# Attention on 128 partitions of four tokens and 32 of two: 1024-byte loads, turns of two tokens of a head, half-height score tiles and three softmax steps

## The reference

```python
# q, k, v: (4, 8, 576, 64)   p: (4, 8, 32, 64)
def sm_attn(qq, kk, vv):
    s = scale * np.matmul(qq, kk.transpose(0, 1, 3, 2))
    s = s - np.max(s, axis=-1, keepdims=True)
    a = np.exp(s)
    a = a / (np.sum(a, axis=-1, keepdims=True) + 1e-09)
    return np.matmul(a, vv)
p_packed = sm_attn(p, k, v)
out = sm_attn(q, p_packed, p_packed)
# then x = out as (2304 tokens, 512); P = gates of x; sum over 8 experts e of
# P[:, e] * (relu(x @ w1[e]) @ w2[e]); then (s * relu(x @ w_in)**2 + b) @ w_out
```

## Time and profile before

| what | value |
|---|---|
| median of 3 runs | 1773.75 us (1773.04 to 1774.57) |
| the profiled execution's own time | 1773.09 us |
| its span, first to last instruction | 1771.1 us |
| PE busy, weight loads busy | 1745.2 us (99%), 1519.9 us (86%) |
| DVE, ACT, POOL busy | 931.5 (53%), 723.1 (41%), 624.2 (35%) us |
| granted TensorE clock | full in all 40 slices |
| DMA, share of 16 engines in the first two slices of 44 us | 90%, 60% |

### The profile page before, as it was taken

How to read it: one execution, slowest core, us unless ns; L and a number is a source line. 1 busy time by engine, 2 the same in 40 slices (tenths; PEclk the granted TensorE clock), 3 DMA queues, 4 the chain that set the end, 5 groups by cost and what they waited for, 6 DMA issues and landing times.

```text
span 1771.1 us, 26764 instructions
## 1 busy us (share of the span) xinstructions
PE 1745.2 (99%) x9861; PEld 1519.9 (86%) x9861; DVE 931.5 (53%) x1441; ACT 723.1 (41%) x1606; POOL 624.2 (35%) x400
## 2 busy tenths in 40 slices
PE   7899999999999999999999999999999999999999
PEld 5688888888898889888988898888888888888887
DVE  5755654445544554554445445544556555555555
ACT  4564446444344434543454444344432322222222
POOL 1364434434544444344444443444431011111100
PEclk9999999999999999999999999999999999999999
DMA  9611112111111211111112111111100000000002
GB/s 231 158 49 36 36 47 50 36 48 36 36 36 36 57 38 40 43 36 36 36 38 57 36 47 36 36 36 36 48 24 24 13 24 25 24 24 24 0 0 107
DMA packets 97294, 78.50 MB, mean 44 GB/s; under 512 B 43744, under 2 KB 84704, under 8 KB 97248
## 3 DMA queue, kind: packets, MB, share of 16 engines
q1 hardware_dynamic: 97248, 77.89, 17.3%
HBM read 73.16 MB, written 4.72 MB: 44 GB/s over the span
## 4 chain that ended last, share of the span: by engine, by line
PE 95%; DVE 2%; ACT 1%; SPq 1%; DMA 0%; issue 0%; DVEq 0%
PE PS L1122 94%; PE PS L1140 1%; DVE acc L978 1%; SPq L362 0%; PE PS L1378 0%; DMA k_raw<-k_dram 0%; DVE gate L955 0%; ACT first_raw L547 0%; DVE a_parts L858 0%; ACT a_parts L547 0%; ACT second L547 0%; DVE stat L809 0%; DVE gate L941 0%; DVE pp L823 0%; DVE stat L834 0%
## 5 line engine op out<-in xcount | busy, mean ns | idle before, releaser
L1122 PE MATMUL PS<-w_hi,h_hi 128*128 128x512 f32 x1440 | 563.6, 391 | 1.2 <-DVE acc L978 1.2
L1122 PE MATMUL PS<-w_hi,h_lo 128*128 128x512 f32 x1440 | 561.0, 390 | 0.0
L1122 PE MATMUL PS<-w_lo,h_hi 128*128 128x512 f32 x1440 | 560.7, 389 | 0.0
L983 DVE SCALAR_TENSOR_TENSOR acc<-PS,gate,acc 128x512 f32<-128x512 f32 x504 | 377.9, 750 | 267.2 <-PE PS L1122 266.6
L684 ACT ACTIVATE h_hi<-PS 128x576 fp32r<-128x576 f32 x256 | 166.9, 652 | 674.2 <-PE PS L1122 673.5
L1122 PE MATMUL PS<-a_parts,g_parts 128*128 128x288 f32 x3072 | 438.3, 295 | 0.8 <-DVE h_lo L964 0.5
L1122 PEld LDWEIGHTS PS<-a_parts,g_parts 128*128 128x128 f32 x3072 | 419.4, 188 | 6.1 <-DVE h_lo L964 1.1
L547 ACT ACTIVATE g_raw<-PS 32x256 f32<-32x256 f32 x992 | 372.3, 375 | 14.2 <-PE PS L1122 0.3
L964 DVE SCALAR_TENSOR_TENSOR h_lo<-PS,h_hi 128x576 fp32r<-128x576 f32 x256 | 193.9, 757 | 325.9 <-ACT h_hi L684 325.9
L1122 PEld LDWEIGHTS PS<-w_hi,h_lo 128*128 128x128 f32 x1440 | 270.3, 188 | 57.8
L1122 PEld LDWEIGHTS PS<-w_hi,h_hi 128*128 128x128 f32 x1440 | 270.4, 188 | 57.3 <-DVE acc L978 3.7
(11 more groups left out here) (129 smaller groups left out, 1107.6 us busy)
## 6 DMA issues: line engine op xcount, KB each, us to landing
stage<-moe_w_dram SPq DMA_DIRECT2D x96, 512.0 KB, 5.1
out_dram<-acc SPq DMA_DIRECT2D x18, 256.0 KB, 2.0
k_raw<-k_dram SPq DMA_DIRECT2D x16, 256.0 KB, 4.5
q_raw<-q_dram SPq DMA_DIRECT2D x16, 256.0 KB, 4.6
v_raw<-v_dram SPq DMA_DIRECT2D x4, 1024.0 KB, 6.1
stage<-moe_w_in_dram SPq DMA_DIRECT2D x16, 256.0 KB, 2.8
stage<-moe_w_out_dram SPq DMA_DIRECT2D x8, 512.0 KB, 3.5
k_tail<-k_dram SPq DMA_DIRECT2D x4, 128.0 KB, 3.9
```

Of the source, the lines that this page charges most:

```text
L983: return nc.vector.scalar_tensor_tensor(out=dst, in0=y, scalar=share, in1=dst, op0=ALU.mult, op1=ALU.add)
L1122: return nc.tensor.matmul(dst, lhsT, rhs, start=start, stop=stop)
```

## The change

Tokens lie otherwise. `main` still has 512 tokens on 128 partitions, four each, but stored by head (`[P, H, 4 * D]`), and `tail` has 64 tokens on 32 partitions, two each. A DMA fetches four heads (a quad) of `main` in pieces of 1024 bytes, and one DMA the tail in pieces of 512 bytes: three DMAs for each of q, k and v. The packed queries are loaded twice side by side (`p_twice`, 256-byte pieces, per batch), which replaces the masks and `queries_by_head`.

A turn takes two tokens of one head (128 columns), so a column of kT or qT has one token in rows 0 to 63 and the next token in rows 64 to 127. k and q take six units each in place of five (for each quad two of four 128x128 turns and one of four 32x128 turns). `CHUNKS` become three: 256, 256 and 64 tokens (128, 128 and 32 columns). The products work on half the array's rows with no zero blocks: `scores1` has 8 products of 64 rows x 32 columns with 288 moving columns in place of 4; `scores2` has 16 products of 64 rows x 128 columns with 32 moving columns per chunk, into two neighbouring PSUM banks, one for each token of a pair; `packed` has 48 products in place of 40, the last 16 on 32 rows; `packed_gates` 8 in place of 4. `scores2` has one pair of banks for all chunks of the first three batches (before: two banks in turn), so a chunk waits until the one before it is taken.

Each step of the second softmax works on 512 elements a partition in place of 256, three times in place of five. `turn_a` makes 512 contiguous columns, and the tokens stay in this order to the end; the output DMAs pick the rows of DRAM, with a stride of four (or two) rows: 24 DMAs in place of 18, unrolled; the last tile is one DMA. `normalise1` writes 128 columns in place of 256 a quad and `pp` needs two turns in place of four, `pp_parts` one copy in place of four, `lo_of_packed` one instruction in place of four. The masks' preparation goes. Batch 0 has an order of its own: its first scores need one quad of k alone, and its packed results come before the turns of batch 1. In the loop k(b+2) and p(b+2) are loaded before v(b+1), and the first expert weights one batch later.

The last piece of the diff is the order of DVE in batches 1 and 2.

```diff
-    MAIN = 512
-    TAIL = S - MAIN
-    CHUNKS = [(c * P, P) for c in range(CH)] + [(MAIN, TAIL)]
+    RUN = 4
+    MAIN = P * RUN
+    TAIL = (S - MAIN) // 2
+    CHUNKS = [(0, P), (P, P), (2 * P, TAIL)]
...
-        LAST_TR, LAST_S2B = (5, 4, 3, 2, 5), (4, 5, 7, 6, 4)
+        LAST_TR, LAST_S2B = (5, 4, 3), (4, 6, 4)
...
+            order = parts("k", 0, range(3)) + parts("p", 0, [0]) + parts("k", 0, range(3, 6)) + parts("q", 0, range(6))
+            order += parts("e", 0, range(3)) + parts("pp", 0, [0]) + parts("p", 1, [0])
+            order += parts("k", 1, range(6)) + parts("q", 1, range(6))
...
         def s2_bank(b, c):
-            return LAST_S2B[c] if b == B - 1 else S2B + (b * NC + c) % 2
+            return LAST_S2B[c] if b == B - 1 else S2B
...
+            def load_quad(dst, src, Q, arrived):
+                sp.dma_start(dst[0][:, Q * 4:Q * 4 + 4, :],
+                             src[Q * 4:Q * 4 + 4, 0:MAIN, :].rearrange("h (p c) d -> p h (c d)", c=RUN)
+                             ).then_inc(arrived, 16)
+
+            def load_tail(dst, src, arrived):
+                sp.dma_start(dst[1][:], src[:, MAIN:S, :].rearrange("h (p c) d -> p h (c d)", c=2)
+                             ).then_inc(arrived, 16)
...
-                sp.wait_ge(tr_full, UNITS.index(("q", b, NC - 1)) + 1)
-                load(q_raw, 0, q, q_in, b + 1)
+                sp.wait_ge(tr_full, UNITS.index(("q", b, UNITS_IN - 1)) + 1)
+                load(q_raw[0], q[b + 1], q_in)
+                if b + 2 < B:
+                    load_queries(b + 2)
+                    load(k_raw[b % 2], k[b + 2], k_in[b % 2])
                 sp.wait_ge(pp_full, b + 1)
-                load_values(b + 1)
+                load(v_raw, v[b + 1], [v_in, v_in, v_in])
...
-                for o in range(2):
-                    lhsT, kk = pT[i][:, Q, o * HALF:(o + 1) * HALF], kT[i][:, 2 * Q + o, :]
-                    mm(bank(S1B)[o * HALF:(o + 1) * HALF, :], lhsT, kk[:, 0:MAIN])
-                    last = mm(bank(S1B + 1, TAIL)[o * HALF:(o + 1) * HALF, :], lhsT, kk[:, MAIN:S])
+                for hq in range(4):
+                    h, out_rows = 4 * Q + hq, slice(hq * NPACK, (hq + 1) * NPACK)
+                    for r in range(2):
+                        rows = slice(r * HALF, (r + 1) * HALF)
+                        last = mm(bank(S1B + r, SPAN)[out_rows, :], pT[i][rows, h * NPACK:(h + 1) * NPACK],
+                                  kT[i][rows, h, :])
...
-                for Q in range(QUADS):
-                    for o in range(2):
-                        last = mm(bank(s2_bank(b, c))[0:rows, Q * P:(Q + 1) * P],
-                                  qT[i][:, 2 * Q + o, col:col + rows], ppT[i][:, 2 * Q + o, :], o == 0, o == 1)
+                for h in range(H):
+                    for r in range(2):
+                        rows = slice(r * HALF, (r + 1) * HALF)
+                        at = (s2_bank(b, c) + r) * BANK + (1 - r) * (BANK - H * NPACK) + h * NPACK
+                        last = mm(PS[0:tokens, at:at + NPACK], qT[i][rows, h, col:col + tokens],
+                                  ppT[i][rows, h * NPACK:(h + 1) * NPACK])
...
+                inverse1(b)
+                inverse2(b - 1, 2)
                 a_chunk(b - 1, 0)
...
                 off_max2(b, 0)
                 max1(b + 1, 0)
+                lo_of_packed(b)
+                inverse2(b, 0)
                 off_max2(b, 1)
+                max1(b + 1, 1)
+                inverse2(b, 1)
+                gates_of_packed(b)
+                off_max2(b, 2)
```

More of the change, by code:

```diff
@@ L357, in load @@
[L357 to L366, removed]
@@ L646, in _ @@
-            for b in range(B):
-                i = b % 2
-                evacuate("e", b, 0, e1T[i][:, 0:CH, 0:P], chunks)
+            for n in range(1, UNITS_IN):
+                q_part(0, n)
+            evacuate("e", 0, 0, *turned_e(0, 0))
+            evacuate("e", 0, 2, *turned_e(0, 2))
+            packed_values(0)
+            p_part(1)
+            exp2(0, 0)
+            k_part(1, 0)
+            k_part(1, 2)
+            exp2(0, 1)
+            exp1(1, 0)
+            k_part(1, 4)
@@ L649, in _ @@
+            k_part(1, 5)
+            exp2(0, 2)
+            q_part(1, 0)
+            exp1(1, 1)
+            for n in range(1, UNITS_IN):
+                q_part(1, n)
+            for b in range(1, B):
+                evacuate("e", b, 0, *turned_e(b, 0))
                 a_chunk(b - 1, 0)
@@ L693, in _ @@
             shift_first(2, 1, 0)
-            for c in range(4):
+            for c in range(2):
                 exp2(B - 1, c)
             relu(0, 0, 0, 0)
-            exp2(B - 1, 4)
+            exp2(B - 1, 2)
             shift_first(3, 0, 1, range(0, 4))
@@ L704, in _ @@
             a_chunk(B - 1, 0)
[L705 to L707 removed]
+            a_chunk(B - 1, 1)
+            shift_products(1, 0, range(0, 4))
+            a_chunk(B - 1, 2)
+            shift_products(1, 0, range(4, SHIFTS))
             for n in range(2 * B):
@@ L890, in _ @@
             k_part(0, 1)
-            dve.wait_ge(p_in, 16)
-            queries_by_head(0)
+            max1(0, 0)
             k_part(0, 3)
-            queries_by_head(1)
-            max1(0, 0)
             max1(0, 1)
-            for b in range(B):
+            inverse1(0)
+            evacuate("e", 0, 1, *turned_e(0, 1))
+            normalise1(0)
+            off_max2(0, 0)
+            k_part(1, 1)
+            inverse2(0, 0)
+            off_max2(0, 1)
+            max1(1, 0)
+            k_part(1, 3)
+            lo_of_packed(0)
+            inverse2(0, 1)
+            off_max2(0, 2)
+            dve.wait_ge(wg_ready, 2)
+            gates_of_packed(0)
+            max1(1, 1)
+            for b in range(1, B):
                 inverse1(b)
+                inverse2(b - 1, 2)
                 a_chunk(b - 1, 0)
-                evacuate("e", b, 1, e1T[b % 2][:, 0:CH, P:2 * P], chunks)
+                evacuate("e", b, 1, *turned_e(b, 1))
                 a_chunk(b - 1, 1)
-                inverse2(b - 1, 4)
                 a_chunk(b - 1, 2)
@@ L1413, in _ @@
                 scores2(last_batch, c)
-            pe.wait_ge(s2_taken, batches + 3)
+            pe.wait_ge(s2_taken, batches + 2)
             packed_gates(last_batch)
```

468 lines of the change are left out of this document (230 added, 238 removed).

## The result

The changed kernel takes 1793.01 us (median of 4, 1787.41 to 1794.29) against 1773.39 us (1772.83 to 1774.57) for the kernel before: ratio 1.0104, 95% interval 1.0082 to 1.0126. I had forecast 1770.4 us and a range from 1765 to 1778. The span grows from 1771.1 to 1790.8 us, +19.7.

The account below looks back on a forecast made before the run. Outside attention PE bounds the kernel; in the attention, 0 to 96 us, no engine is full. Stage terms -5.4 + 4.4 - 1.9 + 0.7 - 1.1 gave -3.3 us, a forecast median of 1770.4 us, range 1765 to 1778.

Parts of the forecast that it names:

- mode changes, packets and VectorE: Named ways to be wrong: array shape changes above 0.17 us each, 1024-byte packets starting later, VectorE held by POOL's longer normalise2.
- To scores2(0, 0): Start to batch 0's first scores2: earlier first scores and shorter preparation, 20.5 us in place of 25.93, -5.4.
- To e(1): From scores2(0, 0) to batch 1's first turn of e: DVE takes all in one line, 14.9 us for 10.47, +4.4.
- the line of DVE steps: Batch 0 to batch 1's turn of e: off_max2, inverse2, copies, maxima and low parts queue on DVE from 22.6 to 33.0 us.
- The middle batches: Batches 1 and 2, between first turns of e: 19.7 and 21.4 us, together 41.1 in place of 43.0, -1.9.
- To the first expert product: From batch 3's first turn of e: eight copies and two off_max2 before packed_gates, 17.0 us for 16.3, +0.7.
- After it: After the first expert product: three turns of a in the last batch, gate_logits no longer waits 1.12 us, -1.1.
- The price of scores2: scores2 per 256 tokens: 32 loads side by side in two row halves, 1.78 us, as much as two chunks before.
- my 0.51: scores1 after the change: 0.51 us if all eight tiles work at once, 1.02 if four; 0.95 before.
- the 350 expected: Loads in the first 16 us: 1024-byte pieces should move near 350 GB/s in the profile after.
- The stall of the earlier trace: Small low parts took 2.12 us beside POOL subtraction, 0.74 elsewhere; laid out it does not recur, 1.4 us gained on top.
- my -3.3: Whole kernel: the sum of the stage changes, taking the span to 1767.8 us.

Follow-up runs that it names:

- g5: Changed kernel with scores2 streaming up to 128 columns a pass and a few long unread products, mostly in PE's waits: 1772.6 us, ratio 0.9992.
- h1: Kernel before, with scores2 of batches 1 and 2 streaming 32 of 128 columns a pass, part of the computation left out: 1774.7 us.
- h2: Kernel before, with scores2 of batches 1 and 2 streaming 32 of 128 columns and scores1 of batches 2 and 3 256 of 512: 1775.6 us.
- g2: Changed kernel with scores2 streaming up to 128 columns a pass behind the same 32 weight loads: 1780.5 us.
- f4: Changed kernel with the eight heads of one row half of scores2 before the eight of the other: 1809.5 us, ratio 1.0187.
- f3: Kernel before with 17 unread 128-column products at the start, 14 before the first turn and 3 before the first scores: 1773.9 us, ratio 0.9999.
- f2: Changed kernel with 14 unread 128-column products before the first turn and 3 before the first scores, none after: 1786.1 us.

## Why the prediction was wrong

My sum had no term for the clock. It took every length of PE at 2.4 GHz, as the rows of the kernel before showed it, and among what "would make me wrong" I named mode changes, packets and VectorE, and not a fall of the clock. That is the step that failed: a term put at nothing without a reason. By the spans of the change and of g5 (1790.8 and 1769.3 us) it is worth 21.5 us. Step by step, forecast, the change, and g5, in which the clock is held:

| stage | forecast | the change | clock held (g5) |
|---|---|---|---|
| start to s2(0, 0) | 20.5 | 23.90 | 21.51 |
| to e(1) | 14.9 | 19.17 | 14.99 |
| to e(2) | 19.7 | 20.15 | 20.49 |
| to e(3) | 21.4 | 29.53 | 21.22 |
| to the first expert product | 17.0 | 21.35 | 16.96 |
| to the end of the span | 1674.3 | 1676.7 | 1674.1 |

1. **To scores2(0, 0), -5.4.** Measured -2.0, and -4.4 with an early rise. PE stayed at 1.2 GHz to 17.32 us, and in the profile of the kernel before, from which my lengths come, to 8.07. How much of this the change makes is open: here 8 turns of k are followed by a tail and a thin `scores1`, where 16 followed each other, but h1 and h2, with the start of the kernel before, rose as late as 16.4 and 16.2 us and lost only 0.9 us by it. The rest, 1.0 us in g5, holds its unread products and the waits for the tail.
2. **To e(1), +4.4.** 14.99 us with the clock held, and 15.03 in g2: the line of DVE steps was right to 0.1 us. The change lost 4.3 us more, with 13.7 us of it at 1.2 GHz.
3. **The middle batches, -1.9.** 41.7 us in g5 for my 41.1, 49.7 in the change. In the second of them each us at 1.2 GHz cost 8.1 / 20.8 = 0.39 us: not one half, since DVE and ACT set part of the pace.
4. **To the first expert product, +0.7.** 16.96 for 17.0; the change lost 4.4 us more.
5. **After it, -1.1.** 1674.1 for 1675.4 in the kernel before, so -1.3. In the change the clock is down to 119.72, and 2.4 us are lost.
6. **The price of scores2, 1.78 us.** 1.97 us in the row, end of the last pass included, and 1.91 to the next start. Right, and f4 shows on what it hangs. `scores1` took 0.65 us to the next start for my 0.51; loads ran at 346 to 362 GB/s in the fullest windows of 2 us up to 22 us, near the 350 expected and below the 378 of the earlier trace rows.
7. **The stall of the earlier trace rows** did not come back: the four low parts of the packed results take 0.42 us each. The three of batches 0 to 2 (36.3, 57.8 and 83.1 us) run while POOL stands idle, as laid out, and the fourth beside a POOL multiplication; what one beside a POOL subtraction would cost is not shown.

The misses of the stages above forecast are 3.4 + 4.3 + 0.5 + 8.1 + 4.4 + 2.4 = 23 us; with my -3.3 they give the +19.7 of the span. g5's span, 1769.3, is 1.5 above the 1767.8 that I laid out, and its median is 1772.6: the forecast's 1770.4 would have been 2 us low with the clock held. g5 also pays for its unread products, so this is what the new attention reached here, and not its floor. So the gain that was there, about 1 us in a median, is at the limit of what can be told from no change, and the clock turned it into a loss of 20.

The lead was in my own working. The changed `scores2` has the same pace as before, set by its loads, while each pass multiplies a quarter of the columns on half the rows, in twice as many passes. I booked that as "no cost". The Trainium skill, "TensorE: Matmul & The Clock Gate", HAM oscillation — how this bites in real kernels, tells of a kernel whose clock falls at each long wait for data. f3 agrees: its clock fell behind a window in which PE waited 1.8 us for a load and was busy for 1.20 of 3.20 us. Other runs go beyond it: g2 took no wait away and won 12.5 us, and h2, whose code adds none, ran at a mean clock of 0.991 to 0.998.

What stays open: the share of each narrow part. `scores2` accounts for 37 of 58 us by one profile of g2 against one of the change, and profiles of one kernel can differ, as f2, h1 and h2 show. `packed` with its 32-row tails, `scores1` on an eighth of the array and the waits at the turns of a were only covered up together (g5), not undone one by one. That code loads cause the "issue" waits of 0.6 to 2.6 us is read from their place beside such loads, and was not tested by itself.

## What to carry to other kernels

A rewrite that leaves PE's time alone but lets it multiply less can cost more than it saves: look at the granted clock first, and before the change ask which stretches will be thin, at the start above all. Where weight loads set the pace, try wider passes: here they were free and worth 12.5 us. When a median has a wide spread, put each run's time beside its mean clock before explaining it in another way, and keep passes on different row halves alternating.

## What the runs showed of the hardware

- In the changed kernel the clock fell behind stretches in which PE was busy for 66 to 87%, with no wait above 1.1 us, and came back by itself; a stretch at 1.2 GHz cost 0.3 to 0.4 us per us in the attention.
- Mean clock orders the times: 1.27 us for 0.001 over 14 runs of two kernels.
- Two row halves run side by side only when neighbouring passes alternate: 1.97 against 3.33 us for 32 passes at 2.4 GHz, 3.43 to 3.63 against 6.17 to 6.21 at 1.2. This is in line with the Trainium skill, "TensorEngine Tiling (Array Packing)", Key Properties, which has tiles load and multiply in parallel; the page's rule says nothing of the order, which f4 shows to decide.
- 32 or 128 columns behind a 128-column load cost the same, 1.97 and 1.98 us for 32 passes.
- POOL's multiplication of 512 elements takes 1.05 us in most rows on 128 partitions and 1.04 on 32.
- The same first 30 us of instructions came to 2.4 GHz at 8.07 us in one profile and at 16.4 and 16.2 us in two others, and `scores2(0, 0)` began 0.9 us later there.
